# The order of the ten output products of a half step, with each narrow product in front of a main one

## The chip, the cores and the metric

The kernel runs on one core of a Trainium2 chip. The metric is device time in microseconds (us), the median of several executions. A profile of one further execution gives spans, busy shares and a timeline.

## The reference

A convolution with softmax weights, and behind it a feed-forward layer with a gate:

```python
w = softmax(weight_gen, axis=-1)              # (4, 4096, 8 heads, 7 taps)
x = sum of 7 shifted rows of x times w        # (4, 4096, 192), per head of 24 channels
h = x.reshape(16384, 192) @ w_in              # (192, 2048)
g = where(h >= 1, h, where(h <= -1, 0, (h + 1)**2 / 4))
out = g @ w_out                               # (2048, 192)
```

## The kernel before

The 16384 tokens are worked in 32 groups of 512. For each group DVE, ACT and POOL make the convolved input one group ahead; TensorE (PE) then makes 16 hidden tiles of 128 features by 512 tokens, ACT and DVE turn each into a gate, and PE multiplies the gates by `w_out`.

Each operand is split into a high and a low part (fp32r), and each product into high by high, low by high and high by low. Input channels are laid out so that a product has 64 rows. A product on partitions 0 to 63 (`LOWER`) and one on 64 to 127 (`UPPER`) can run side by side in the two halves of the array.

**Hidden products.** `hidden_unit(pair, b, n, j)` is product j of 9 for hidden tile n, L997 in the profile. Even tiles lie in the lower half, odd ones in the upper.

**Output products.** A half step k covers tiles 2k and 2k+1, and has one side for the lower 64 features of each and one for the upper 64. `out_unit(pair, b, k, side, i)` is product i of 10 of a side. Six are main products (L1023): for each tile high, part (the low part of the weights) and low (the low part of the gate), summed in `acc_main`, output channels 0 to 127. Four are rest products (L1037) summed in `acc_rest`: for each tile one wide, 128 columns (the 64 other channels by both parts of the weights), and one narrow, 64 columns. Before, their order is: high, part, low of the first tile, the same of the second, then wide, narrow, wide, narrow. In the last side of a group the second tile's two rest products stand in reverse: wide, narrow, narrow, wide.

**The queue.** `tile_pair` writes PE's order out by hand, alternating between the halves, 19 products in each:

```python
for i in range(UNITS + OUT_UNITS):
    if i < UNITS: hidden_unit(pair, b, 2 * k, i)
    else:         out_unit(*lower, 0, i - UNITS)
    if i < OUT_UNITS: out_unit(*upper, 1, i)
    else:             hidden_unit(pair, b, 2 * k + 1, i - OUT_UNITS)
```

`lower` is the half step two tile pairs back (`LAG = 2`), `upper` the one three back. There are 256 tile pairs, 8 in a group; the first three are written apart, and the tail after the last one finishes the last half steps, at its end with products of all 128 rows (`last_rest`, L1047 to L1050, and `last_main`, L1056 to L1058).

**Waits of PE.** `outputs_ready` waits until the low part of a tile's gate is there (`gate_low_done`). Both halves add into the same accumulators, so a side's first main product waits until the other half's last main product of the side before has ended (`main_side_done`), and its first rest product for the last rest product (`rest_side_done`). DVE transposes the accumulators of a finished group (`turn_out_rest`, `turn_out_main`) during the next group's tiles 5 and 6, and SyncE stores them.

Of the kernel before, what the change touches and what calls it, by code (L numbers as in the profile page):

```python
# [21 lines left out]
GATES = 8  # L22
# [17 lines left out]
FIRST_TILES = 4  # L40
FIRST_UNITS, FIRST_LAST_UNITS = (0, 1, 3, 4, 2, 6, 7), (5, 8)
FIRST_FILLS = (4, 5)
QUADS = 4
LANES = P // QUADS
MAIN = 32
# [6 lines left out]
def build(nc, x, weight_gen, w_in, w_out, out):  # L52
# [4 lines left out]
    NT = FF // P  # L57
# [6 lines left out]
    PAD = K - 1  # L64
    CH = D // QUADS
    HQ = H // QUADS
    REST = CH - MAIN
# [6 lines left out]
    SIDE = D - P  # L74
    UNITS = 9
    OUT_UNITS = 10
    OUT_MAINS = 6
    assert P == QUADS * MAIN and 2 * REST == MAIN and H % QUADS == 0 and S % RUN == 0 and RUN % (2 * STEP) == 0
    assert NT % W_CHUNKS == 0 and NT % GATES == 0 and NT % SLOTS == 0


    x_quads = (x.rearrange("b s d -> (b s d)").rearrange("(r t d) -> r t d", r=LANES, d=D)
               .rearrange("r t (q c) -> q r t c", q=QUADS))
    w_quads = (weight_gen.rearrange("b s h k -> (b s h k)").rearrange("(r t e) -> r t e", r=LANES, e=H * K)
               .rearrange("r t (q e) -> q r t e", q=QUADS))
    out_lanes = (out.rearrange("t d -> (t d)").rearrange("(r t d) -> r t d", r=LANES, d=D)
# [4 lines left out]
    with ExitStack() as ctx:  # L91
        def sb(name, shape, dt=F32):
            return ctx.enter_context(nc.sbuf_tensor(name, shape, dt))

        def sem(name):
            return ctx.enter_context(nc.semaphore(name))
# [33 lines left out]
        out_w_main = sb("out_w_main", [P, NT, 2, P], F32R)  # L130
# [4 lines left out]
        gate_high = [sb(f"gate_high{b}", [P, GT], F32R) for b in range(GATES)]  # L135
        gate_low = [sb(f"gate_low{b}", [P, GT], F32R) for b in range(GATES)]
# [4 lines left out]
        acc_main = [ctx.enter_context(nc.psum_tensor(f"acc_main{b}", [P, GT], F32)) for b in range(2)]  # L141
        acc_rest = [ctx.enter_context(nc.psum_tensor(f"acc_rest{b}", [P, GT], F32)) for b in range(2)]
# [50 lines left out]
        main_side_done = sem("main_side_done")  # L193
        rest_side_done = sem("rest_side_done")
        upper_copied = sem("upper_copied")
        last_summed = sem("last_summed")
        out_main_turned = sem("out_main_turned")
        out_rest_turned = sem("out_rest_turned")
# [5 lines left out]
        def wait(eng, semaphore, pair, per_pair, offset):  # L204

            if isinstance(pair, int):
                if per_pair * pair + offset > 0:
                    eng.wait_ge(semaphore, per_pair * pair + offset)
            else:
                eng.wait_ge(semaphore, pair * per_pair + offset)  # L210
# [8 lines left out]
        def is_first(pair):  # L219
            return isinstance(pair, int) and pair == 0  # L220
# [19 lines left out]
        SIDES = 2 * NP  # L240
# [727 lines left out]
        def _(pe):  # L968
# [33 lines left out]
            def outputs_ready(pair, b, n):  # L1002

                wait(pe, gate_low_done, pair, 2 * NT, NT * b + n + 1)
                if b == 0 and is_first(pair) and n % CT == 0:
                    pe.wait_ge(out_low_done, n // CT + 1)

            def both_sides(n):
                return out_w_side[:, n, :, :].rearrange("p a d -> p (a d)")

            def out_unit(pair, b, k, side, i):

                rows, turn = (LOWER, UPPER)[side], 2 * k + side
                if i < OUT_MAINS:
                    n, j = 2 * k + i // 3, i % 3
                    if i % 3 == 0 and side == 0:
                        outputs_ready(pair, b, n)
                    if i == 0 and turn == 0:
                        wait(pe, out_main_turned, pair, 2, b - 1)
                    elif i == 0:  # L1020
                        wait(pe, main_side_done, pair, 2 * SIDES, SIDES * b + turn)
                    gate = (gate_low if j == 2 else gate_high)[n % GATES]
                    ins = nc.tensor.matmul(acc_main[b][:], out_w_main[rows, n, 1 if j == 1 else 0, :], gate[rows, :],  # L1023
                                           start=(turn == 0 and i == 0), stop=(turn == SIDES - 1 and i == OUT_MAINS - 1))
                    if i == OUT_MAINS - 1:
                        ins.then_inc(main_side_done, 1)
                else:
                    n, j = 2 * k + (i - OUT_MAINS) // 2, i % 2
                    if i == OUT_MAINS and turn == 0:
                        wait(pe, out_rest_turned, pair, 2, b - 1)  # L1030
                    elif i == OUT_MAINS:
                        wait(pe, rest_side_done, pair, 2 * SIDES, SIDES * b + turn)
                    wide = j == 0 if turn < SIDES - 1 or n < NT - 1 else j == 1
                    to = acc_rest[b][:] if wide else acc_rest[b][0:SIDE, :]
                    w = both_sides(n)[rows, :] if wide else out_w_side[rows, n, 0, :]
                    gate = (gate_high if wide else gate_low)[n % GATES]
                    ins = nc.tensor.matmul(to, w, gate[rows, :], start=(turn == 0 and i == OUT_MAINS),  # L1037
                                           stop=(turn == SIDES - 1 and i == OUT_UNITS - 1))
                    if i == OUT_UNITS - 1:
                        ins.then_inc(rest_side_done, 1)  # L1040

            def last_rest(n):
# [40 lines left out]
            def warm(count, bank=slot[0]):  # L1083
                for i in range(count):
                    nc.tensor.matmul(bank[:, 0:P], ident[:], ident[:], start=True, stop=True)
# [19 lines left out]
                for n in (FIRST_TILES, FIRST_TILES + 1):  # L1105
                    hidden_unit(0, 0, n, j)
            for i in range(OUT_UNITS):
                if i in (0, OUT_MAINS // 2):
                    warm(FIRST_FILLS[i // (OUT_MAINS // 2)], acc_rest[0])
                out_unit(0, 0, 0, 0, i)  # L1110

            def tile_pair(pair, b, k):

                lower = (pair, b, k - LAG) if k >= LAG else (*before(pair, b), NP + k - LAG)
                upper = (pair, b, k - LAG - 1) if k > LAG else (*before(pair, b), NP + k - LAG - 1)
                for i in range(UNITS + OUT_UNITS):
                    if i < UNITS:
                        hidden_unit(pair, b, 2 * k, i)
                    else:
                        out_unit(*lower, 0, i - UNITS)  # L1120
                    if i < OUT_UNITS:
                        out_unit(*upper, 1, i)
                    else:
                        hidden_unit(pair, b, 2 * k + 1, i - OUT_UNITS)
# [37 lines left out]
```

## Time and profile before

| | us |
|---|---|
| median of 3 executions | 1143.71 (1142.37 to 1143.74) |
| the profiled execution | 1143.08 |
| its span | 1141.5 |
| PE busy | 1130.2 (99%), 9790 products |
| loads of weights (PEld) busy | 1093.0 (96%) |
| DVE, ACT, POOL busy | 790.4, 884.6, 811.4 |

Matmuls are pipelined: one is in the trace for some 387 ns, and the next of its half starts before it ends. What counts is the distance between starts. PEld overlaps PE.

### The profile page before, as it was taken

What the parts mean: (1) busy time and instruction counts of PE and PEld (TensorE: products, weight loads), DVE (VectorE), ACT (ScalarE), POOL (GpSimd) and SP (SyncE); (2) the same over time, 40 slices, a digit from 0 to 9 for tenths busy, and PEclk for the clock granted to TensorE, in tenths of its full rate; (3) what the DMA queues carried; (4) which work ended last, traced back from release to release, by engine and by line L of the source; (5) the groups of instructions that cost most, each with busy time, mean ns of one, the idle gap of its engine ahead of it and who ended that gap; (6) DMA issues with size and microseconds to landing.
All of it is one profiled execution on the core that took longest, in us unless ns stands there. A gap on an engine that the chain in (4) does not pass through costs nothing.

```text
span 1141.5 us, 28171 instructions
## 1 busy us (share of the span) xinstructions
PE 1130.2 (99%) x9790; PEld 1093.0 (96%) x9790; DVE 790.4 (69%) x1280; ACT 884.6 (77%) x1655; POOL 811.4 (71%) x579
## 2 busy tenths in 40 slices
PE   8999999999999999999999999999999999999998
PEld 7789999999999999999999999999999999999997
DVE  6866676776677776677766677766677766777665
ACT  4877777777778777887777878777887778877775
POOL 6688876667876668866678766678766688676610
PEclk9999999999999999999999999999999999999999
DMA  8323334223344223343223342233442233442111
GB/s 156 83 50 64 71 74 78 59 52 60 64 78 78 55 40 68 71 78 75 51 44 69 74 78 59 53 59 64 78 78 56 42 68 69 78 77 51 20 47 29
DMA packets 287257, 74.15 MB, mean 65 GB/s; under 512 B 266304, under 2 KB 268352, under 8 KB 287232
## 3 DMA queue, kind: packets, MB, share of 16 engines
q1 hardware_dynamic: 280784, 72.92, 33.0%
q10 hardware_dynamic: 6448, 0.90, 0.6%
q8 instruction: 15, 0.25, 0.1%
q14 instruction: 10, 0.08, 0.0%
HBM read 24.10 MB, written 12.58 MB: 32 GB/s over the span
## 4 chain that ended last, share of the span: by engine, by line
PE 95%; DVE 1%; SPq 1%; DMA 1%; ACT 1%; issue 0%; POOL 0%; ACTq 0%; DVEq 0%
PE slot L997 48%; PE acc_main L1023 28%; PE acc_rest L1037 19%; SPq L351 0%; DMA x_in<-in_x 0%; DMA xt_swap_low<-xt_low 0%; DMA xt_side_low<-rest_turn 0%; SPq L339 0%; ACT square L677 0%; DVE taps_all L460 0%; ACT gate_high L682 0%; DVE gate_low L813 0%; DVE slot L807 0%; SPq L387 0%; ACT half_relu L671 0%
## 5 line engine op out<-in xcount | busy, mean ns | idle before, releaser
L1023 PE MATMUL acc_main<-gate_high,out_w_main 64*128 64x512 f32 x2032 | 623.9, 387 | 0.0
L813 DVE TENSOR_TENSOR gate_low<-slot,gate_high 128x512 fp32r<-128x512 f32 x510 | 352.9, 692 | 334.9 <-ACT gate_high L682 329.9
L671 ACT ACTIVATE half_relu<-slot 128x512 f32<-128x512 f32 x510 | 304.2, 597 | 186.3 <-PE slot L997 182.8
L1037 PE MATMUL acc_rest<-gate_low,out_w_side 64*64 64x512 f32 x1016 | 394.7, 393 | 0.0
L1023 PE MATMUL acc_main<-gate_low,out_w_main 64*128 64x512 f32 x1016 | 392.7, 386 | 0.0
L1037 PE MATMUL acc_rest<-gate_high,out_w_side 64*128 64x512 f32 x1016 | 392.1, 386 | 0.0
L1023 PEld LDWEIGHTS acc_main<-gate_high,out_w_main 64*128 64x128 f32 x2032 | 374.2, 184 | 3.7
L807 DVE SCALAR_TENSOR_TENSOR slot<-slot,square 128x512 f32<-128x512 f32 x510 | 350.5, 687 | 2.8 <-ACT square L677 2.8
L682 ACT ACTIVATE gate_high<-slot 128x512 fp32r<-128x512 f32 x510 | 304.6, 597 | 49.4 <-DVE slot L807 44.5
L677 ACT ACTIVATE square<-half_relu 128x512 f32<-128x512 f32 x512 | 321.5, 628 | 0.0
L460 POOL TENSOR_TENSOR taps_all<-x_in,tap_w 128x768 f32<-128x768 f32 x188 | 289.5, 1548 | 0.0
L488 POOL TENSOR_TENSOR conv<-conv,taps_all 128x768 f32<-128x768 f32 x120 | 222.3, 1853 | 0.0
L997 PE MATMUL slot<-xt_high,in_high 64*128 64x512 f32 x510 | 198.6, 391 | 0.4 <-issue 0.4
L997 PE MATMUL slot<-xt_swap_low,in_high 64*128 64x512 f32 x510 | 196.2, 386 | 2.3 <-DMA xt_swap_low<-xt_low 2.3
L997 PE MATMUL slot<-xt_side_high,in_high 64*128 64x512 f32 x510 | 196.2, 387 | 1.3 <-DMA xt_side_high<-rest_turn 1.3
L997 PE MATMUL slot<-xt_side_low,in_high 64*128 64x512 f32 x510 | 196.6, 387 | 0.2 <-DMA xt_side_low<-rest_turn 0.2
L997 PE MATMUL slot<-xt_high,in_low 64*128 64x512 f32 x510 | 196.5, 387 | 0.0
L997 PE MATMUL slot<-xt_swap_high,in_high 64*128 64x512 f32 x510 | 196.4, 387 | 0.0
L997 PE MATMUL slot<-xt_low,in_high 64*128 64x512 f32 x510 | 196.2, 387 | 0.0
L997 PE MATMUL slot<-xt_side_high,in_low 64*128 64x512 f32 x510 | 196.2, 387 | 0.0
L997 PE MATMUL slot<-xt_swap_high,in_low 64*128 64x512 f32 x510 | 196.1, 386 | 0.0
L1037 PEld LDWEIGHTS acc_rest<-gate_high,out_w_side 64*128 64x128 f32 x1016 | 187.5, 185 | 0.9
(142 smaller groups left out, 1742.3 us busy)
## 6 DMA issues: line engine op xcount, KB each, us to landing
x_in<-in_x SPq DMA_DIRECT2D x122, 132.0 KB, 3.0
out<-taps_all SPq DMA_DIRECT2D x189, 64.0 KB, 1.8
xt_side_high<-rest_turn SPq DMA_DIRECT2D x64, 128.0 KB, 3.1
xt_side_low<-rest_turn SPq DMA_DIRECT2D x64, 128.0 KB, 3.2
xt_swap_high<-xt_high SPq DMA_DIRECT2D x62, 128.0 KB, 2.5
xt_swap_low<-xt_low SPq DMA_DIRECT2D x62, 128.0 KB, 2.9
taps_all<-taps_all SPq DMA_DIRECT2D x31, 128.0 KB, 2.2
gen_in<-in_weight_gen SPq DMA_DIRECT2D x122, 28.0 KB, 2.0
```

The costliest lines, as they stand in the source:

```text
L460: return ops.tensor_tensor((dst if isinstance(dst, bass.AP) else dst[:]).rearrange("p t (h c) -> p t h c", h=HQ), x_in[b][:, k:k + STEP, : ...
L488: nc.gpsimd.tensor_tensor(to[:], conv[b][:], tap[k % 3][:], ALU.add).then_inc(conv_step, 1)
L671: nc.scalar.activation(half_relu[n % 2][:], tile_slot(pair, b, n)[:], ACT.Relu, scale=0.5, bias=0.5).then_inc(relu_done, 1)
L677: nc.scalar.activation(square[n % 2][:], half_relu[n % 2][:], ACT.Square).then_inc(square_done, 1)
L682: nc.scalar.activation(gate_high[n % GATES][:], tile_slot(pair, b, n)[:], ACT.Copy).then_inc(gate_high_done, 1)
L807: nc.vector.scalar_tensor_tensor(h[:], h[:], 1.0, square[n % 2][:], ALU.max, ALU.min).then_inc(gate_done, 1)
L813: nc.vector.tensor_tensor(gate_low[n % GATES][:], tile_slot(pair, b, n)[:], gate_high[n % GATES][:].bitcast(F32), ALU.subtract).then_inc(g ...
L997: ins = nc.tensor.matmul(tile_slot(pair, b, n)[:], w[rows, part, at:at + P], xt[b][rows, :], start=(j == 0), stop=(j == UNITS - 1))
L1023: ins = nc.tensor.matmul(acc_main[b][:], out_w_main[rows, n, 1 if j == 1 else 0, :], gate[rows, :], start=(turn == 0 and i == 0), stop=(tu ...
L1037: ins = nc.tensor.matmul(to, w, gate[rows, :], start=(turn == 0 and i == OUT_MAINS), stop=(turn == SIDES - 1 and i == OUT_UNITS - 1))
```

## The change

The ten products of a side get an order written in a table, one for the lower and one for the upper side. The first lower side of the kernel keeps the order of before. Number, operands and accumulators of the products stay; a side's first main and first rest product carry the waits as before, and each tile's gate is waited for at the first product of that tile.

```diff
+OUT_ORDERS = (((0, "wide"), (1, "wide"), (0, "narrow"), (0, "high"), (0, "part"), (0, "low"),
+               (1, "high"), (1, "narrow"), (1, "part"), (1, "low")),
+              ((0, "wide"), (0, "narrow"), (0, "high"), (0, "part"), (0, "low"),
+               (1, "wide"), (1, "narrow"), (1, "high"), (1, "part"), (1, "low")))
+FIRST_OUT_ORDER = ((0, "high"), (0, "part"), (0, "low"), (1, "high"), (1, "part"), (1, "low"),
+                   (0, "wide"), (0, "narrow"), (1, "wide"), (1, "narrow"))
...
-            def out_unit(pair, b, k, side, i):
+            def out_unit(pair, b, k, side, i, order=None):
...
-                if i < OUT_MAINS:
-                    n, j = 2 * k + i // 3, i % 3
-                    if i % 3 == 0 and side == 0:
-                        outputs_ready(pair, b, n)
+                order = OUT_ORDERS[side] if order is None else order
+                half, kind = order[i]
+                n, final = 2 * k + half, turn == SIDES - 1
+                main = kind in ("high", "part", "low")
+                same = [at for at in range(OUT_UNITS) if (order[at][1] in ("high", "part", "low")) == main]
+                if side == 0 and i == [at for at, _ in order].index(half):
+                    outputs_ready(pair, b, n)
+                if main:
+                    if i == same[0]:
+                        if turn == 0:
+                            wait(pe, out_main_turned, pair, 2, b - 1)
+                        else:
+                            wait(pe, main_side_done, pair, 2 * SIDES, SIDES * b + turn)
...
-                    wide = j == 0 if turn < SIDES - 1 or n < NT - 1 else j == 1
+                    if i == same[0]:
+                        if turn == 0:
+                            wait(pe, out_rest_turned, pair, 2, b - 1)
+                        else:
+                            wait(pe, rest_side_done, pair, 2 * SIDES, SIDES * b + turn)
+                    wide = (kind == "wide") != (final and half == 1)
...
-                out_unit(0, 0, 0, 0, i)
+                if FIRST_OUT_ORDER[i][1] == "high":
+                    warm(FIRST_FILLS[FIRST_OUT_ORDER[i][0]], acc_rest[0])
+                out_unit(0, 0, 0, 0, i, FIRST_OUT_ORDER)
```

## Rows read from the trace of the kernel before

**Rows 1.** The page: busy time, share of the span, instructions of each engine.

```profile
PE 1130.2 (99%) x9790; PEld 1093.0 (96%) x9790; DVE 790.4 (69%) x1280; ACT 884.6 (77%) x1655; POOL 811.4 (71%) x579
```

**Rows 2.** The page: the chain that ended last, by engine.

```profile
PE 95%; DVE 1%; SPq 1%; DMA 1%; ACT 1%; issue 0%; POOL 0%; ACTq 0%; DVEq 0%
```

**Rows 3.** Busy time by stage: stage, its length, engines, PEclk, DMA share, GB/s.

```profile
60.00:600.00 540.00, 540.00 (x4745) 527.41 (x4743) 376.24 (x610) 424.63 (x797) 407.77 (x285) 1.00 0.33 63
```

**Rows 4.** Groups of loads by shape: count, busy us, mean ns, idle before.

```profile
L1037 PEld LDWEIGHTS acc_rest<-gate_high,out_w_side 64*128 64x128 f32 x1016 | 187.5, 185 | 0.9
...
L1037 PEld LDWEIGHTS acc_rest<-gate_low,out_w_side 64*64 64x64 f32 x1016 | 133.2, 131 | 1.0
```

**Rows 5.** Timeline of PE, steady part, lower half: start us, us, engine, line.

```profile
553.36 0.39 PE L997 MATMUL slot<-xt_high,in_high 64*128 64x512 f32 x1
...
557.71 0.39 PE L997 MATMUL slot<-xt_high,in_high 64*128 64x512 f32 x1
...
601.21 0.39 PE L997 MATMUL slot<-xt_high,in_low 64*128 64x512 f32 x1
...
604.38 0.39 PE L1037 MATMUL acc_rest<-gate_high,out_w_side 64*128 64x512 f32 x1
...
605.31 0.39 PE L997 MATMUL slot<-xt_high,in_high 64*128 64x512 f32 x1
```

**Rows 6.** Timeline of PE in the tail, products of 128 rows.

```profile
1132.84 0.39 PE L1047 MATMUL acc_rest<-gate_high,out_w_side 128*128 128x512 f32 x1
1133.07 0.40 PE L1048 MATMUL acc_rest<-gate_low,out_w_side 128*64 128x512 f32 x1
...
1134.00 0.39 PE L1047 MATMUL acc_rest<-gate_high,out_w_side 128*128 128x512 f32 x1
...
1136.07 0.39 PE L1058 MATMUL acc_main<-gate_low,out_w_main 128*128 128x512 f32 x1
```

**Rows 7.** Timeline of PE, upper half, last side of a group (one of 31).

```profile
550.79 0.39 PE L1037 MATMUL acc_rest<-gate_low,out_w_side 64*64 64x512 f32 x1
...
551.03 0.39 PE L1037 MATMUL acc_rest<-gate_low,out_w_side 64*64 64x512 f32 x1
...
552.64 0.39 PE L997 MATMUL slot<-xt_swap_low,in_high 64*128 64x512 f32 x1
```

**Rows 8.** Timeline of PE and of its loads, around a lower side's first main product.

```profile
554.68 0.39 PE L1023 MATMUL acc_main<-gate_low,out_w_main 64*128 64x512 f32 x1
...
555.18 0.18 PEld L1023 LDWEIGHTS acc_main<-gate_high,out_w_main 64*128 64x128 f32 x1
```

**Rows 9.** Timeline, all engines: a load that waits, and an ACT instruction that waits.

```profile
44.23 0.68 DVE L813 TENSOR_TENSOR gate_low<-slot,gate_high 128x512 fp32r<-128x512 f32 x1
...
44.96 0.18 PEld L997 LDWEIGHTS slot<-xt_high,in_high 64*128 64x128 f32 x1 [0.29 <-DVE gate_low L813]
...
45.07 0.19 PEld L997 LDWEIGHTS slot<-xt_high,in_low 64*128 64x128 f32 x1
...
600.93 0.39 PE L997 MATMUL slot<-xt_side_low,in_high 64*128 64x512 f32 x1
...
601.35 0.60 ACT L671 ACTIVATE half_relu<-slot 128x512 f32<-128x512 f32 x1 [0.29 <-PE slot L997]
```

**Rows 10.** Timeline, all engines: first group, a group's end, a gate.

```profile
29.14 0.40 PE L1037 MATMUL acc_rest<-gate_low,out_w_side 64*64 64x512 f32 x1
...
29.32 0.18 PEld L1023 LDWEIGHTS acc_main<-gate_high,out_w_main 64*128 64x128 f32 x1
...
44.49 0.18 PEld L1023 LDWEIGHTS acc_main<-gate_high,out_w_main 64*128 64x128 f32 x1
...
516.63 0.38 PE L1037 MATMUL acc_rest<-gate_high,out_w_side 64*128 64x512 f32 x1
...
523.42 0.71 DVE L863 STREAM_TRANSPOSE taps_all<-acc_main 128x512 f32<-128x512 f32 x1
...
600.58 0.69 DVE L813 TENSOR_TENSOR gate_low<-slot,gate_high 128x512 fp32r<-128x512 f32 x1
```

More of the change, by code:

```diff
@@ L76, in build @@
     OUT_UNITS = 10
-    OUT_MAINS = 6
     assert P == QUADS * MAIN and 2 * REST == MAIN and H % QUADS == 0 and S % RUN == 0 and RUN % (2 * STEP) == 0
@@ L1009, in both_sides @@
                 return out_w_side[:, n, :, :].rearrange("p a d -> p (a d)")
-            def out_unit(pair, b, k, side, i):
+            def out_unit(pair, b, k, side, i, order=None):
                 rows, turn = (LOWER, UPPER)[side], 2 * k + side
-                if i < OUT_MAINS:
-                    n, j = 2 * k + i // 3, i % 3
-                    if i % 3 == 0 and side == 0:
-                        outputs_ready(pair, b, n)
[L1018 to L1025, printed above, removed]
+                order = OUT_ORDERS[side] if order is None else order
[11 more added lines that the diff above has]
+                            wait(pe, main_side_done, pair, 2 * SIDES, SIDES * b + turn)
+                    gate = (gate_low if kind == "low" else gate_high)[n % GATES]
+                    ins = nc.tensor.matmul(acc_main[b][:], out_w_main[rows, n, 1 if kind == "part" else 0, :],
+                                           gate[rows, :], start=(turn == 0 and i == same[0]),
+                                           stop=(final and i == same[-1]))
+                    if i == same[-1]:
@@ L1026, in out_unit @@
                         ins.then_inc(main_side_done, 1)
                 else:
[L1028 to L1032, printed above, removed]
-                    wide = j == 0 if turn < SIDES - 1 or n < NT - 1 else j == 1
+                    if i == same[0]:
[3 more added lines that the diff above has]
+                            wait(pe, rest_side_done, pair, 2 * SIDES, SIDES * b + turn)
@@ L1036, in out_unit @@
                     gate = (gate_high if wide else gate_low)[n % GATES]
-                    ins = nc.tensor.matmul(to, w, gate[rows, :], start=(turn == 0 and i == OUT_MAINS),
-                                           stop=(turn == SIDES - 1 and i == OUT_UNITS - 1))
-                    if i == OUT_UNITS - 1:
+                    ins = nc.tensor.matmul(to, w, gate[rows, :], start=(turn == 0 and i == same[0]),
+                                           stop=(final and i == same[-1]))
+                    if i == same[-1]:
                         ins.then_inc(rest_side_done, 1)
@@ L1107, in _ @@
             for i in range(OUT_UNITS):
-                if i in (0, OUT_MAINS // 2):
-                    warm(FIRST_FILLS[i // (OUT_MAINS // 2)], acc_rest[0])
-                out_unit(0, 0, 0, 0, i)
+                if FIRST_OUT_ORDER[i][1] == "high":
+                    warm(FIRST_FILLS[FIRST_OUT_ORDER[i][0]], acc_rest[0])
+                out_unit(0, 0, 0, 0, i, FIRST_OUT_ORDER)
             def tile_pair(pair, b, k):
```

## The prediction

> **What bounds the kernel now.** I first read the busy shares: PE 99%, no other engine over 77% [rows 1], and the chain of waits, 95% PE [rows 2]. By stage, PE is busy all of 60 to 600 us at full clock, 1.00 of the 2.4 GHz level [rows 3]. So a change can only act through how fast PE takes its queue. DVE, ACT, POOL and the DMAs are cover, unless PE comes to wait for them.
>
> Then I read PE's timeline. The lower half (partitions 0 to 63) and the upper half of the array each take 19 products per tile pair; I number them places 0 to 18. Lower: 0 to 8 hidden, 9 to 18 output. Upper: 0 to 9 output, 10 to 18 hidden. Eleven tile pairs, from 557.71 to 605.31, take 47.60 us, 4.327 each [rows 5]. In the lower half, places 1 to 15 are 14 steps without a narrow product: 601.21 to 604.38, 3.17 us [rows 5]. The rounding allows 0.2261 to 0.2271 a step and I take 0.2267. Nineteen such steps would be 4.307. So the two narrow products of a half step cost that half 4.327 - 4.307 = **0.020 us**, lost in the five steps behind them. Both halves lose it at their own places, in the same 4.327. A narrow load is shorter, 131 against 184 ns, but both fit under a step of 227 ns [rows 4], so its shortness earns nothing; its neighbourhood costs.
>
> **The change, part by part.**
>
> *Products and loads.* Nothing is added or removed: ten products a half step, two of them narrow, the same weights and sides. Only places move. The first lower half step (FIRST_OUT_ORDER) keeps its order.
>
> *Spacing of the narrow products.* Before, they stand two places apart (lower 16 and 18, upper 7 and 9), both with rest products around them. After, five apart (lower 11 and 16, upper 1 and 6), each with a main product behind. What is a lone narrow product worth? The tail shows one: rest wide at 1132.84, narrow at 1133.07, three main products, the next wide at 1134.00, 1.16 us for five steps that should be 5 x 0.2267 = 1.133 [rows 6]. That is the whole 0.02 again, for one narrow product, and it is the very order of the new upper side. Two directly adjacent cost more: in the tail 1134.00 to 1136.07 is 2.07 for nine steps (2.040), 0.03 [rows 6]; in the steady part, at the last half step of a group, 550.79 to 552.64 is 1.85 for eight steps (1.814), 0.03 to 0.04 [rows 7]. So PE stumbles for some five steps after a narrow load, about 0.020; a second one two places on falls into the running stumble and is free; one place on it adds 0.013. Five places apart, each starts its own. The tail is in 128-row form, but the adjacent case costs the same in both forms, so I carry it over. Bounds: 0 (the second is still free) to 0.020 extra. I take 0.020 per tile pair. The two halves stumble side by side, so it counts once.
>
> *PE's waits for itself.* A side may start on an accumulator only when the other half's side has ended. The smallest distance, last product of a side to first of the next, was four places (upper main 5 to lower main 9); after, it is three in all four cases (upper 6 to lower 9, upper 9 to lower 12, lower 16 to upper 0, lower 18 to upper 2). Normally a load starts with the product before its own, two places after the product waited for: 0.453 us, less the lag of the upper half behind the lower where the lower waits, plus it where the upper waits. What the wait needs: a product's end is known about 0.40 after its start (ACT starts 0.42 after one, 600.93 to 601.35), and a load that waits starts about 0.05 after the release (gate_low ends 44.23 + 0.68, load 44.96) [rows 9], so 0.45. Where a second wait stands in the queue (the gates of the tile: lower place 9), the trace's shortest distance is 0.50: product at 554.68, load at 555.18 [rows 8]. The product before it starts in that same 0.01 us, so the load was hardly late, and still the tile pair lasted 557.71 - 553.36 = 4.35 instead of 4.33 [rows 5]. Nine tile pairs, sixteen apart, do this (about 0.2 us in all). So I price a late load at 0.02 to 0.03, say 0.027. After the change lower place 9 needs 0.50 and has 0.453 minus the lag: late in every tile pair. Upper place 9's load stands behind it in the queue and is late by about 0.05 whatever the lag. Products themselves need not stop: a product can follow its load by 0.11 (load at 44.96, the next at 45.07 when its product had begun [rows 9]), which leaves 0.227 - 0.11 = 0.12 of slack; a lag over about 0.06 (0.12 - 0.05) costs the lower half time until it has shrunk. For the lower half the late load merges with the stumble of place 11 (adjacent case: 0.03 to 0.04 for that, then place 16 falls inside it: still about 0.04 in all). For the upper half it falls into the stumble of place 6: between 0 (free, as a second narrow product two places on) and 0.027 (full, as at 555.18). I take 0.013, the price of a disturbance close to another one.
>
> *Gates.* The odd tile of a half step is needed at place 10, not 12. In a steady tile pair its gate_low ends at 600.58 + 0.69 = 601.27 [rows 10] and the load would start at place 9, 601.21 + 8 x 0.2267 = 603.02: 1.75 of cover. Only in the first group is it short: the load at 44.49 [rows 10] would be the odd tile's and wait until 44.96, 0.47; of that PE already loses about 0.25 now, a hidden product's load waiting for the same gate (idle 0.29 [rows 9]): 0.22 more. And the first upper side now waits for the narrow product at 29.14 [rows 10]: its load can start 0.45 later, 29.59, against 29.32 now [rows 10], 0.27. Together 0.5, once; without any cover 0.7.
>
> *DVE.* The group's rest accumulator is finished three places earlier, the main one four places (0.9 us) later. DVE turns the main one at 523.42, when the side's last product of before had started at 516.63 [rows 10]; 0.2 us later than that is still over 6 us ahead. Covered. Stores and copies follow DVE, unmoved.
>
> *Sum.* Per tile pair 0.020 + 0.013, less 0.001 for the nine late loads of before, now contained: 0.032. Times 253 tile pairs: 8.0 us. With 0.5 at the start, the profiled execution's 1143.08 (span 1141.5 and 1.6 around it) becomes **1151.6**. That execution stands 0.63 below the median of 1143.71, 0.05%, so I leave it out.
>
> *A rule that points elsewhere.* In the rows a lone narrow product, with two changes between 64 and 128 columns, costs 0.02, and an adjacent pair, also with two, 0.03 to 0.04 [rows 6, 7]. The Trainium skill, TensorEngine Tiling (Array Packing), Key Properties, says that changing the tiling mode drains the engine; by it the price would hang on the number of changes, four a half step before and four after, and the sum would be 0. The adjacent pair's row speaks against it.
>
> **Rivals.**
> *Loads never late enough to matter* (0.22). If the second wait costs nothing after all, only the spacing counts: 0.020 x 253 = 5.1, with 0.5: 1148.6.
> *The price is per change of shape* (0.11): each time a product of 64 columns and one of 128 follow each other costs 0.005, four times per half step before and after, so nothing changes: 1143.1 to 1143.6 with the start. For it: two narrow products cost 0.020. Against it: the lone one in the tail costs as much.
> *The waits stop products* (0.13). If a late load costs a full restart in both halves, or both can't be served at one lag, two of the four waits cost 0.027 to 0.05 each beyond the spacing: 0.05 to 0.10 a pair, 1157 to 1170. Against: the needs (0.50 and 0.45) sum to 0.95 against 0.91 given, a shortfall of 0.04 that the 0.12 slack of a product covers.
> *Faster: a narrow product costs only before another product on the same accumulator* (0.13). Before, narrow at 16 is followed by a wide rest product. If a main product behind it, in another bank, frees it, both stumbles vanish: 253 x 0.020 = 5.1, less 0.5 at the start: 1138.5. It decides if the price of a narrow product before a main one is under 0.010. Against: in the tail narrow is followed by main and still costs 0.02, one sample.
> The forecast itself: 0.41; its own range is 0 to 0.027 for the late load: 1148.3 to 1155.5.
>
> **How the numbers follow.** Forecast, first rival and most of the stopping one lie at 1148 and above, the shape rival at 1143.5. 1143.5 to 1161 leaves out the faster case and the far end of the stopping one, about 0.2. 0.2% is 2.3 us, about what a measurement tells from no change. Slower: 0.41 + 0.22 + 0.13 = 0.76; same: 0.11; faster: 0.13.
>
> **What the profile would show.** Right: tile pairs of 4.35 to 4.37; in the upper half, place 0 to 5 and 5 to 10 each 1.15 to 1.17; lower place 9's load 0.50 after upper place 6's product, later than the product before its own; a lag of the upper half below 0.07; loads before lone narrow products in their usual place. Wrong: tile pairs of 4.31 (faster rival), 4.33 (shape), over 4.38 with gaps at places 9, 12, 0 or 2 (stopping). What would make it wrong most easily is a late load that is free inside a running stumble, or one that costs more when it is 0.05 rather than some ns late.

## The result and the profile after

The changed kernel takes 1151.29 us (median of 4 executions, 1150.33 to 1152.15), the kernel before 1143.72 on the same chip: ratio 1.0070, 95% interval 1.0058 to 1.0083. It is slower, by 7.6 us; forecast were 1151.6 and slower.

The page of the changed kernel and its stage from 60 to 600 us, to be read beside [rows 1 to 3]:

```profile
PE 1138.1 (99%) x9790; PEld 1078.0 (94%) x9790; DVE 790.3 (69%) x1280; ACT 871.3 (76%) x1655; POOL 811.2 (71%) x579
```

```profile
PE 95%; DVE 1%; SPq 1%; DMA 1%; ACT 1%; issue 0%; POOL 0%; ACTq 0%; DVEq 0%
```

```profile
60.00:600.00 540.00, 540.00 (x4705) 510.03 (x4705) 371.57 (x602) 415.14 (x787) 406.68 (x283) 1.00 0.33 63
```

PE's shares hide the change. PE is busy 99% as before, at the same clock, the chain is PE's at 95% as before. In the stage two numbers move. In the same 540 us PE starts 4705 products, 40 fewer than the 4745 of before [rows 3], 0.8%: that is the loss. Its loads are busy 510.03 us instead of 527.41, which is no gain: the loads of the two halves lie closer together and cover each other more.

The timeline of PE (start us, us, engine, line) says where. Three times the hidden product at lower place 0: of the seventh tile pair after the three that are written apart, and of two that are eight tile pairs apart:

```profile
60.62 0.39 PE L1002 MATMUL slot<-xt_high,in_high 64*128 64x512 f32 x1
...
492.46 0.39 PE L1002 MATMUL slot<-xt_high,in_high 64*128 64x512 f32 x1
...
527.37 0.39 PE L1002 MATMUL slot<-xt_high,in_high 64*128 64x512 f32 x1
```

A tile pair takes (527.37 - 492.46) / 8 = 4.364 us, before 4.327 [rows 5]. In the kernel before, the product of the first of these rows stands here:

```profile
60.09 0.39 PE L997 MATMUL slot<-xt_high,in_high 64*128 64x512 f32 x1
```

So 0.53 us are lost by then, over six tile pairs. The rest is 0.035 a tile pair, 8.6 over the other 247. Together 9.1, the difference of the two profiled spans being 1150.5 - 1141.5 = 9.0.

The 0.53 is not all the new order's. One tile pair earlier, at lower place 0, it is 51.61 - 51.38 = 0.23. Then both kernels wait 2.7 us for the same DMA (before and after):

```profile
51.38 0.39 PE L997 MATMUL slot<-xt_high,in_high 64*128 64x512 f32 x1
...
55.04 0.18 PEld L997 LDWEIGHTS slot<-xt_swap_low,in_high 64*128 64x128 f32 x1 [2.68 <-DMA xt_swap_low<-xt_low]
```

```profile
51.61 0.39 PE L1002 MATMUL slot<-xt_high,in_high 64*128 64x512 f32 x1
...
55.20 0.18 PEld L1002 LDWEIGHTS slot<-xt_swap_low,in_high 64*128 64x128 f32 x1 [2.67 <-DMA xt_swap_low<-xt_low]
```

PE goes on 0.16 later than before. Soon after, the granted clock stands at 0.50, the 1.2 GHz level, for 3.4 us in both profiled executions (stages, before and after):

```profile
55.48:58.88 3.40, 3.40 (x18) 2.27 (x16) 1.27 (x4) 1.61 (x3) 2.48 (x3) 0.50 0.75 96
```

```profile
56.75:60.15 3.40, 3.40 (x20) 2.61 (x18) 1.30 (x2) 1.61 (x3) 3.16 (x4) 0.50 0.93 152
```

The changed kernel has this stretch 1.3 us later, and by its end the 0.16 has become 0.53. The traces of other runs (the earlier gate wait, for one) have the DMA wait without such a stretch; what decides it no run shows.

Now one tile pair, upper half: places 0, 5, 10 and 15, then place 0 of the next tile pair and of the one after it.

```profile
549.26 0.39 PE L1048 MATMUL acc_rest<-gate_high,out_w_side 64*128 64x512 f32 x1
...
550.41 0.39 PE L1048 MATMUL acc_rest<-gate_high,out_w_side 64*128 64x512 f32 x1
...
551.57 0.39 PE L1002 MATMUL slot<-xt_high,in_high 64*128 64x512 f32 x1
...
552.72 0.39 PE L1002 MATMUL slot<-xt_swap_low,in_high 64*128 64x512 f32 x1
...
553.63 0.39 PE L1048 MATMUL acc_rest<-gate_high,out_w_side 64*128 64x512 f32 x1
...
557.97 0.39 PE L1048 MATMUL acc_rest<-gate_high,out_w_side 64*128 64x512 f32 x1
```

Five steps of 0.2267 would be 1.133. The first five take 1.15, the second 1.16, the third 1.15: three stumbles of 0.02 one behind another. The last four take 0.91, the undisturbed 0.907. Two stumbles are the narrow products at places 1 and 6. The third follows place 9, where there is none. The cause is in the loads of the same tile pair (PE and PEld rows in order of time: upper 6, lower 8, upper 8, the loads of lower 9 and upper 9, then lower 9, the load of lower 10, and lower 10):

```profile
550.64 0.39 PE L1048 MATMUL acc_rest<-gate_low,out_w_side 64*64 64x512 f32 x1
...
551.00 0.39 PE L1002 MATMUL slot<-xt_side_low,in_high 64*128 64x512 f32 x1
...
551.10 0.39 PE L1033 MATMUL acc_main<-gate_high,out_w_main 64*128 64x512 f32 x1
...
551.15 0.18 PEld L1048 LDWEIGHTS acc_rest<-gate_high,out_w_side 64*128 64x128 f32 x1
551.18 0.18 PEld L1033 LDWEIGHTS acc_main<-gate_low,out_w_main 64*128 64x128 f32 x1
...
551.23 0.42 PE L1048 MATMUL acc_rest<-gate_high,out_w_side 64*128 64x512 f32 x1
551.28 0.18 PEld L1048 LDWEIGHTS acc_rest<-gate_high,out_w_side 64*128 64x128 f32 x1
...
551.49 0.39 PE L1048 MATMUL acc_rest<-gate_high,out_w_side 64*128 64x512 f32 x1
```

Lower place 9's load starts at 551.15, 0.51 after upper place 6's product and 0.15 after the product it should start with (551.00). Upper place 9's load stands behind it in the queue and starts 0.08 after its own (551.10). Lower place 9 is on record for 0.42 instead of 0.39, and the last row, lower place 10, stands 0.49 after place 8 instead of 0.453, so there the lower half stood still for 0.03 to 0.04. In this tile pair the lower half takes 4.39, in the next 4.35: the stop makes the lag of the upper half small, the upper half's extra stumble makes it large again. The upper half's pace is the pair's pace.

The trace holds its own counter-test. In the tile pair from 553.63 to 557.97, 4.35 long, the lower side starts a fresh accumulator and has no side of the upper half to wait for; the load of upper place 9 is in place. Over the 239 tile pairs from some 80 to 1125 us, this load is 0.08 late in 195, and the upper half takes 4.367 in nearly all of them; in the other 44 it is in place, and the upper half takes 4.347. These 44 are the tile pair of the fresh accumulator in each group and, in every other group, the one two ahead of it, where the load of lower place 9 starts 0.45 after upper place 6's product instead of 0.51; why, the traces don't show.

### The profile page after: what moved, and what is told of

Read it like the earlier page. It is cut to its first block, busy times and chain, and to the rows that moved or that the text cites. A ratio compares the mean times of both kernels' runs of the same rounds, so it can differ in the third digit from the quotient of the medians.

```text
span 1150.5 us, 28171 instructions
## 1 busy us (share of the span) xinstructions
PE 1138.1 (99%) x9790; PEld 1078.0 (94%) x9790; DVE 790.3 (69%) x1280; ACT 871.3 (76%) x1655; POOL 811.2 (71%) x579
## 4 chain that ended last, share of the span: by engine, by line
PE 95%; DVE 1%; SPq 1%; DMA 1%; ACT 1%; issue 0%; POOL 0%; ACTq 0%; DVEq 0%
PE slot L1002 45%; PE acc_main L1033 30%; PE acc_rest L1048 19%; DMA xt_side_low<-rest_turn 1%; SPq L356 0%; DMA x_in<-in_x 0%; SPq L344 0%; ACT square L682 0%; DVE taps_all L465 0%; ACT gate_high L687 0%; SPq L392 0%; DVE gate_low L818 0%; DVE slot L812 0%; ACT half_relu L676 0%; ACT in_high L727 0%
## 5 line engine op out<-in xcount | busy, mean ns | idle before, releaser
L1033 PE MATMUL acc_main<-gate_high,out_w_main 64*128 64x512 f32 x2032 | 670.4, 389 | 0.0
L1048 PE MATMUL acc_rest<-gate_low,out_w_side 64*64 64x512 f32 x1016 | 400.0, 394 | 0.0
L1048 PE MATMUL acc_rest<-gate_high,out_w_side 64*128 64x512 f32 x1016 | 356.3, 390 | 0.0
L1048 PEld LDWEIGHTS acc_rest<-gate_high,out_w_side 64*128 64x128 f32 x1016 | 177.1, 184 | 19.9
```

## The experiments

Each was timed on one chip beside the kernel before, in three rounds unless more are named; medians and ratios with 95% intervals are against it. Where two rows of PE's timeline stand, they are lower place 0, 80 tile pairs apart.

**No narrow product, order of before.**

```diff
-                    to = acc_rest[b][:] if wide else acc_rest[b][0:SIDE, :]
-                    w = both_sides(n)[rows, :] if wide else out_w_side[rows, n, 0, :]
+                    to = acc_rest[b][:]
+                    w = both_sides(n)[rows, :]
```

> The kernel before, with each narrow rest product made wide (128 columns; this adds the product of the two low parts, which the reference contains and the kernel before leaves out). Same order, same number of products, longer loads. My theory (a narrow load makes PE stumble for some five steps, 0.020 us a tile pair): the stumbles vanish, tile pairs of 4.307, 1143.7 - 253 x 0.020 = 1138.6. Rival (the loss comes from rest products following each other on one accumulator, or from shape-independent causes): tile pairs stay at 4.327, 1143.7. Rival (a longer load costs): over 1144.

```profile
465.87 0.39 PE L997 MATMUL slot<-xt_high,in_high 64*128 64x512 f32 x1
...
810.40 0.39 PE L997 MATMUL slot<-xt_high,in_high 64*128 64x512 f32 x1
```

344.53 / 80 = 4.307. 1138.52 us, ratio 0.9957 (0.9940 to 0.9974). The loads are longer and the kernel is faster by 5.1: the narrow products' price, all of it.

**One narrow product a side.** As above, but wide only where `wide or n % 2 == 1`.

> The kernel before, with only the second tile's narrow product made wide; the first tile's stays narrow, so one narrow product a side is left, followed by wide ones. My theory: a lone narrow product costs the whole 0.020, the second one two places on was free: tile pairs of 4.327, 1143.7, no change. Rival (each narrow product, or each change between 64 and 128 columns, has its own price, 0.010 or 0.005): tile pairs of 4.317, 1141.2.

```profile
468.49 0.39 PE L997 MATMUL slot<-xt_high,in_high 64*128 64x512 f32 x1
...
814.63 0.39 PE L997 MATMUL slot<-xt_high,in_high 64*128 64x512 f32 x1
```

346.14 / 80 = 4.327, as with two. 1143.24 us, ratio 0.9996 (0.9986 to 1.0006). One narrow product costs what two cost two places apart. Prices per product and per change of shape both fall.

**The two narrow products adjacent.**

```diff
-                    wide = j == 0 if turn < SIDES - 1 or n < NT - 1 else j == 1
+                    wide = j == n % 2
```

> The kernel before, with the rest products of every side as wide, narrow, narrow, wide: the narrow ones directly behind each other, two changes of shape a side instead of four. My theory: 0.033 a tile pair instead of 0.020, so 4.340; 1143.7 + 253 x 0.0133 = 1147.1. Rival (price per change of shape, 0.005): 4.317, 1141.2.

```profile
468.97 0.39 PE L997 MATMUL slot<-xt_high,in_high 64*128 64x512 f32 x1
...
816.16 0.39 PE L997 MATMUL slot<-xt_high,in_high 64*128 64x512 f32 x1
```

347.19 / 80 = 4.340. 1146.41 us, ratio 1.0024 (1.0015 to 1.0034). Half as many changes of shape, and 0.013 a tile pair more. The interval reaches down to 0.15%, but all tile pairs of the steady part take 4.340.

**Changed order, the gate waited for one product earlier.**

```diff
-                if side == 0 and i == [at for at, _ in order].index(half):
+                if side == 0 and (half == 1 or order is FIRST_OUT_ORDER) and i == [at for at, _ in order].index(half):
...
+                    if i == UNITS - 1:
+                        outputs_ready(*lower[:2], 2 * lower[2])
                     if i < UNITS:
                         hidden_unit(pair, b, 2 * k, i)
```

> The changed kernel, with the wait for the even tile's gate (always over there by then) put at the hidden product ahead of lower place 9, so that the first rest product carries one wait only. My theory: its load then starts 0.45 instead of 0.50 after upper place 6's product, the upper load behind it is no longer late, the third stumble of the upper half and the stops of the lower vanish: tile pairs of 4.347 instead of 4.363, 1151.3 - 253 x 0.016 = 1147.3 to 1149. Rival (the lateness comes from the distance of three places, not from the second wait): 1151.

Upper place 6's product, then the loads of lower 9 and upper 9, and the two rows 80 tile pairs apart:

```profile
468.19 0.39 PE L1002 MATMUL slot<-xt_high,in_high 64*128 64x512 f32 x1
...
547.82 0.39 PE L1048 MATMUL acc_rest<-gate_low,out_w_side 64*64 64x512 f32 x1
...
548.27 0.18 PEld L1048 LDWEIGHTS acc_rest<-gate_high,out_w_side 64*128 64x128 f32 x1
548.29 0.18 PEld L1033 LDWEIGHTS acc_main<-gate_low,out_w_main 64*128 64x128 f32 x1
...
815.92 0.39 PE L1002 MATMUL slot<-xt_high,in_high 64*128 64x512 f32 x1
```

The wait now takes 548.27 - 547.82 = 0.45 instead of 0.51, and the upper load is in place again. 347.73 / 80 = 4.347: 4.307 and two stumbles. 1147.79 us, ratio 1.0042 (1.0027 to 1.0056) to the kernel before, 3.5 less than the changed kernel. The loads of lower places 9 and 12 still start 0.02 to 0.03 after the product ahead of them in most tile pairs, without a price beyond the two stumbles. So in this kernel three places are enough for one wait and too few for two.

**Changed order, no narrow product.** The edit of the first experiment in the changed kernel: the late loads alone.

> The changed kernel with both narrow rest products made wide: its order and its waits, but no narrow product, so only the waits three places apart are left. My theory: lower place 9's load and upper place 9's behind it are late in 7 of 8 tile pairs, each a full stumble of 0.020 to 0.027 in its half, side by side: tile pairs of about 4.327, 1138.5 + 0.5 + 253 x 7/8 x 0.022 = 1143.9. Rival (a late load costs only next to a narrow product's stumble): 1139.

```profile
468.22 0.39 PE L1002 MATMUL slot<-xt_high,in_high 64*128 64x512 f32 x1
...
815.33 0.39 PE L1002 MATMUL slot<-xt_high,in_high 64*128 64x512 f32 x1
```

347.11 / 80 = 4.339, so 0.032 a tile pair, more than the 0.022 that I expected: 1145.63 us against 1143.9, ratio 1.0017 (1.0007 to 1.0026). Late loads need no narrow product to cost. Alone they cost 0.032, on top of the two stumbles only 0.017 (4.364 less 4.347), so the costs don't simply add up. Here the price is uneven too: of the 241 tile pairs the upper half takes about 4.32 in nearly half, 4.35 to 4.39 in most others. How the price of one late load depends on how late it is, no run separates.

**Both costs taken away.** The two edits together in the changed kernel.

> The same, with the even tile's gate waited for at the product before, so that no load has two waits: both suspected costs taken away from the changed order. My theory: tile pairs of 4.307, 1138.5 + 0.5 for the start = 1139. If something else in the new order costs time it shows here as more than 1139.5.

```profile
464.54 0.39 PE L1002 MATMUL slot<-xt_high,in_high 64*128 64x512 f32 x1
...
809.19 0.39 PE L1002 MATMUL slot<-xt_high,in_high 64*128 64x512 f32 x1
```

344.65 / 80 = 4.308. 1137.66 us, ratio 0.9950 (0.9934 to 0.9967). Nothing else in the new order costs time.

**96 columns instead of 64.** Order of before, `to = acc_rest[b][0:SIDE * 3 // 2, :]` with the weights to match. Its loads and two rows 80 tile pairs apart:

> The kernel before, with the narrow products widened from 64 to 96 columns (the 32 more add a part of the product of the two low parts; the sum is the reference's to rounding). Is it any shape under 128 columns that makes PE stumble, or is the price in proportion to what is missing? My theory says only that a load of another length disturbs a locked rhythm: the whole 0.020, 1143.7. Rival (in proportion to the columns missing): 0.010, 1141.1. Rival (only the form of 64 columns is special): 1138.6.

```profile
L1037 PEld LDWEIGHTS acc_rest<-gate_low,out_w_side 64*96 64x96 f32 x1016 | 160.8, 158 | 1.4
```

```profile
468.66 0.39 PE L997 MATMUL slot<-xt_high,in_high 64*128 64x512 f32 x1
...
815.06 0.39 PE L997 MATMUL slot<-xt_high,in_high 64*128 64x512 f32 x1
```

346.40 / 80 = 4.330. 1144.25 us, ratio 1.0011 (1.0002 to 1.0021). The load is 26 ns shorter than a wide one's 184 instead of 53, and the price isn't half: it is not in proportion to the columns missing. The 0.003 above 4.327 comes from one tile pair in eight. In the upper half 210 of 240 take 4.327, the same as with 64 columns; the 30 with the last side of a group, where the two stand adjacent, take 4.353, against 4.340 in the kernel before.

**The two fastest side by side, five rounds.**

> The order of before without narrow products, timed again in more rounds beside the next one. My theory: 0.5% faster than the kernel before, tile pairs of 4.307.

> The changed order without narrow products and with the earlier gate wait, beside the one above. My theory: with both costs gone the orders are alike, tile pairs of 4.307, within 1 us of the old order without narrow products. Rival: the new order is better by itself, over 1 us faster than it.

Without narrow products the order of before takes 1136.72 us, ratio 0.9948 (0.9935 to 0.9962); the new order with the earlier gate wait takes 1138.18, ratio 0.9952 (0.9939 to 0.9966). The medians are 1.5 apart, more than the 1 us that I expected, and the new order is the slower one; in the runs of three rounds, on two other chips, it was the other way round, 1137.66 against 1138.52. The steady part is the same, 4.307 in both traces. The profiled execution of the new order has the stretch of 3.4 us at a granted clock of 0.50 (56.2 to 59.6 us), that of the old order has none; a step takes 0.427 us there instead of 0.227, so that 3.4 us do the work of 1.8. So the orders are alike within what this measures. Both beat both kernels, the order of before without narrow products with the smaller edit.

## Why the prediction was right

*Spacing, 0.020 a tile pair.* Right, and shown apart from the waits: 4.347 with the earlier gate wait, 0.020 over the kernel before. The number itself hung on a choice: of steps from 0.2261 to 0.2271 that the rows allow (with both roundings 0.2257 to 0.2271) I took 0.2267, and over 19 steps that range makes the price anything from 0.01 to 0.04. The kernel without narrow products settles it, 4.307 / 19 = 0.2267. The argument rested on one lone narrow product in the tail, in 128-row form [rows 6]; the experiment with one narrow product a side shows it over the whole kernel in 64-row form.

*Late loads, 0.013.* The mechanism was right: the load of lower place 9 at 0.51 (predicted 0.50), the upper one behind it late. The size was low: upper place 9's load is 0.08 late, not 0.05, and costs a third full stumble, 0.020, in that half. In the tile pair of each group in which the lower side starts a fresh accumulator, the lower side doesn't wait for the upper one, and this stumble is absent; over a group it is 4.364 - 4.347 = 0.017. I had counted it in all 253. The two errors half cancel: 0.035 a tile pair against 0.032.

*The stop of products.* I had it as a lag that shrinks once. It comes back: in many tile pairs the lower half stands for 0.03 to 0.04 and catches its lag up again. It costs nothing beyond the upper half's stumbles. The sign that I had named, a lag of the upper half below 0.07, came true in part only: the lag is mostly 0.05 to 0.10, at place 8 of the tile pair shown 551.10 - 551.00 = 0.10.

*Start, 0.5.* The total of 0.53 at 60 us agrees by luck. The wait of the first upper side is there: the narrow product starts at 29.27 and the load at 29.71, 0.44 later (rows below), and the first tile pair behind it takes 0.23 longer than before, forecast 0.27. The 0.22 for the gate isn't there: at 34.15 the kernel is 0.36 behind, at 51.61 only 0.23, and 0.12 of either it had before its first changed product (29.50 against 29.38 for the same hidden product). The rest came with the DMA wait and the stretch at the lower clock, which I hadn't counted.

```profile
29.27 0.39 PE L1048 MATMUL acc_rest<-gate_low,out_w_side 64*64 64x512 f32 x1
...
29.71 0.18 PEld L1048 LDWEIGHTS acc_rest<-gate_high,out_w_side 64*128 64x128 f32 x1
```

*Gates and DVE* cost nothing in the steady part, as forecast: with both costs removed the new order runs at 4.308.

*The sum.* 253 x 0.032 is 8.1, not 8.0, which changes nothing. 1143.08 + 8.0 + 0.5 was made against the profiled execution, whose counterpart took 1152.15: a difference of 9.1, against 8.5 forecast. The medians are 7.6 apart. That 1151.29 agrees with 1151.6 so closely is luck in part: the terms are not that good.

*The rivals.* The price per change of shape is refuted by one narrow product (same time with half the changes) and by the adjacent ones (half the changes, more time). By the rule of the Trainium skill, TensorEngine Tiling (Array Packing), Key Properties, that changing the tiling mode drains the engine, the price would follow the number of changes. Between products of 64 and 128 columns this case shows no such price: 4.327 with two changes a side as with four, 4.340 with two. That loads are never late enough to matter: refuted by the changed order without narrow products. That the waits stop products: the lower half does stop, but the tile pair stays at 4.364, under the 4.38 that I had named for it. Its 1157 to 1170 was added up without the spacing that it was to come on top of; with it, it starts at 1161, the upper end of the range that I gave. 1151.29 is far from both. That a main product behind a narrow one makes it free: refuted, 4.347.

## What to carry to other kernels

When PE starts products back to back, read the distance between starts over a fixed number of places, not the busy share: 99% busy hid both a 0.5% gain and a 0.7% loss. In this stream a product of another width, or a load that starts late though its product is in time, disturbs the rhythm for some five products; disturbances close together can share a price and spread out each pays its own, so keep all products of one shape if the work allows it, and otherwise, as far as this kernel shows, bunch the odd ones two places apart. And before moving a product nearer to the one it waits for, count the waits at that place: a second wait at the same product needed 0.06 us more than a single one (0.51 against 0.45) and delayed what stood behind it in the other half.

## What was unexpected of the hardware

A longer load is the faster one: wide loads of 184 ns throughout give 4.307 us a tile pair, with loads of 131 or 158 ns among them it is 4.327 to 4.330. One load of 131 ns costs 0.020 us, a second one two places on nothing, one place on 0.013.

The stumble has a fixed form. With one narrow product a side, the mean steps over all steady tile pairs are, from the product ahead of it on, 225.8, 235.8, 228.3, 232.5 and 230.8 ns, then 226.7 again. With two of them two places apart they are the same. Directly adjacent ones make it nine steps long: 225.9, 235.8, 229.2, 224.1, 230.9, and then 235.8, 228.3, 232.5, 230.8, the end of a single stumble once more. What in PE makes these slow steps the runs don't show; only what starts them and what doesn't.

The undisturbed step doesn't depend on the lag between the halves: it is 226.7 ns with a lag near 0 (without narrow products) and with 0.14 to 0.16 (mean by place, the kernel before). Where the halves met in these runs was the queue, in which a wait of one half holds the other's load: 0.08 us late behind a double wait, in place behind a single one.
